# Two dense layers after attention: the up projection as seven half-block products over 768 tokens, with streamed weights

## The chip, the cores and the metric

One NeuronCore of a Trainium2 chip runs the program. The metric is the device time of one execution in microseconds (us). The engines are TensorE (PE, its weight loads are PEld), VectorE (DVE), ScalarE (ACT), GpSimd (POOL) and SyncE (SP, which issues the DMAs here).

## The reference

Attention over 4 x 8 heads of 576 positions and width 64 gives `x`, 2304 tokens by 512. It goes through two dense layers, each an up projection to 2048 and a down projection back to 512, all in float32.

```python
out_up = np.repeat(sm_attn(q_d, k_d, v_d), 4, axis=2)      # attention over positions pooled by 4
out_local = softmax(where(|i - j| < 4, scale * q @ k.T, -1e9)) @ v
x = (out_up + out_local)                                   # 2304 x 512
h = x @ w_in;  g = where(h > 0, h, exp(min(h, 0)) - 1);  x = g @ w_out      # first layer
h = x @ w_in;  r = maximum(h, 0);  g = s * (r * r) + b;  out = g @ w_out    # second layer
```

## The kernel before

**Attention** goes over 16 pairs of heads (4 batches of 4), software-pipelined by hand: `pairs()` runs one `step` per pair on each engine. SP loads queries, keys and values (L240 to L255). GpSimd pools queries and values (L356 to L365) and VectorE keys (L674); VectorE masks, takes maxima, and normalises (L681, L715, L723); ScalarE exponentiates (L555, L565) and copies transposed probabilities out of PSUM (L595 to L605). The result lies in `xy`, with the model dimension on partitions in four groups of 128 (`CH`).

**The dense layers.** Every product is made of three passes: each float32 operand is split into a high part (ScalarE, a copy to fp32r) and a low part (the operand minus its high part), and TensorE adds high x high, high x low and low x high. The tokens go in 6 blocks of 384 (`TB`, `NB`), the inner dimension of 2048 in 16 chunks of 128 (`j`). `up(layer, n, j)` makes one chunk of `h` for one block: 4 groups x 3 passes = 12 matmuls of 384 columns into one of four PSUM banks `ps_h` (L504). `down` adds that chunk's part of the block's output into `ps_y`: in the first layer 12 matmuls of 384 columns (L523), in the second, where tokens lie on output partitions, 9 of 512 columns (L525). TensorE runs `up` two chunks ahead of `down`. Per chunk ScalarE and VectorE apply the activation (first layer: L637, L640, L776; second: L637, L780, L782) and split it (L643 high, L784 low). At the end of a block ScalarE and VectorE copy `ps_y` out (L651, L655, L791, L795); the next block's operand is split four pieces at a time (L576, L729).

**The weights** of a layer stay in SBUF, split once per layer: 256 KB pieces come into the two halves of `wstage` (L263), ScalarE makes the high part (L573, `hi_w`), GpSimd the low part (L370, `lo_w`). Four chunks of the first layer (`win_early`, `wout_early`) are loaded and split during attention; the other twelve (`win_late`, `wout_late`) take the place of attention's buffers. The second layer's weights replace the first's during its last block and the second layer's first. The output goes to memory from `wstage` in pieces of 128 tokens (L317).

The order on every engine is written out in the program; semaphores (`g_ready`, `act_ready`, `w_split`, ...) carry the dependences.

## Time and profile before

| | us |
|---|---|
| median of 3 runs (lowest, highest) | 945.64 (943.05, 947.13) |
| profiled execution: its time | 941.55 |
| profiled execution: span, first to last instruction | 939.7 |
| busy: TensorE matmul, weight load | 907.7, 853.8 |
| busy: VectorE, ScalarE, GpSimd | 412.4, 413.3, 154.2 |
| mean granted TensorE clock | 0.987 of 2.4 GHz |

A span is cut into stretches to see which engine fills which. "Busy" sums the time in which at least one instruction of the engine runs; a matmul's length reaches from its start to its modelled end, and the next one starts before that, so the price of a matmul is the distance between starts. The chain of waits follows the work that ended last back in time, and tells which instructions the time consists of.

### The profile page before, as it was taken

Reading aid. Unit: us, or ns where it says so; the run is one execution under the profiler, and the core shown is the slowest. Engines: PE = TensorE matmul, PEld = TensorE weight load, DVE = VectorE, ACT = ScalarE, POOL = GpSimd, SP = SyncE. Lnnn points to the kernel's source line nnn. Section 1 sums busy time; section 2 is a strip of 40 time slices with the busy share of each in tenths; the row PEclk is TensorE's granted clock in tenths of the full one; section 3 lists DMA queues with packets and bytes.
Section 4 is the critical chain, followed back from the end, with each engine's and each line's share of the span. In section 5 each row is a group of like instructions: output and inputs, shape, how many; then the busy total and the mean of one; then the engine's idle time right before and its main releaser. Section 6 shows DMA issues by size and latency. Waiting matters only on the chain.

```text
span 939.7 us, 16134 instructions
## 1 busy us (share of the span) xinstructions
PE 907.7 (97%) x5936; PEld 853.8 (91%) x5936; DVE 412.4 (44%) x773; ACT 413.3 (44%) x1103; POOL 154.2 (16%) x147
## 2 busy tenths in 40 slices
PE   5988889999999999999999999999999999999998
PEld 4777679999999999999999989989999899899996
DVE  5999964333233233233233353443443443443433
ACT  6888887534334344344366532232232232232222
POOL 6565637500000000000056500000000000000000
PEclk9899999999999999999999999999999999999999
DMA  9999915300000000000044300000000000000000
GB/s 179 181 189 180 178 57 146 101 1 1 1 1 0 0 0 0 0 1 1 1 124 124 90 1 1 34 1 1 34 0 0 34 0 0 34 1 0 35 1 34
DMA packets 42929, 41.47 MB, mean 44 GB/s; under 512 B 3616, under 2 KB 30080, under 8 KB 42880
## 3 DMA queue, kind: packets, MB, share of 16 engines
q1 hardware_dynamic: 42880, 40.83, 19.0%
q8 instruction: 30, 0.49, 0.2%
q14 instruction: 19, 0.16, 0.1%
HBM read 36.09 MB, written 4.72 MB: 43 GB/s over the span
## 4 chain that ended last, share of the span: by engine, by line
PE 87%; DVE 3%; SPq 3%; issue 2%; ACT 2%; DMA 1%; POOL 1%; DVEq 0%; ACTq 0%; POOLq 0%
PE ps_h L504 43%; PE ps_y L525 21%; PE ps_y L523 21%; DMA wstage<-in_w_in 1%; SPq L240 1%; SPq L253 1%; ACT prob L555 1%; DVE stat L704 1%; PE ps_t L437 1%; DVE prob L681 1%; DVE xy L764 1%; SPq L249 1%; DVE kd L674 0%; SPq L254 0%; PE ps_s L413 0%
## 5 line engine op out<-in xcount | busy, mean ns | idle before, releaser
L643 ACT ACTIVATE g_hi<-tmp 128x384 fp32r<-128x384 f32 x192 | 101.0, 526 | 261.9 <-PE ps_y L525 152.2
L784 DVE TENSOR_TENSOR g_lo<-tmp,g_hi 128x384 fp32r<-128x384 f32 x192 | 107.3, 559 | 204.7 <-ACT g_hi L643 204.7
L637 ACT ACTIVATE tmp<-ps_h 128x384 f32<-128x384 f32 x192 | 94.3, 491 | 227.7 <-PE ps_h L504 225.3
L504 PE MATMUL ps_h<-xs_hi,win_late_lo 128*128 128x384 f32 x576 | 193.8, 336 | 0.0
L504 PE MATMUL ps_h<-xs_hi,win_late_hi 128*128 128x384 f32 x576 | 193.8, 336 | 0.0
L504 PE MATMUL ps_h<-xs_lo,win_late_hi 128*128 128x384 f32 x576 | 193.6, 336 | 0.0
L776 DVE SCALAR_TENSOR_TENSOR tmp<-tmp,ps_h 128x384 f32<-128x384 f32 x96 | 53.2, 554 | 161.8 <-ACT tmp L640 161.0
L504 PEld LDWEIGHTS ps_h<-xs_lo,win_late_hi 128*128 128x128 f32 x576 | 108.3, 188 | 3.3
L504 PEld LDWEIGHTS ps_h<-xs_hi,win_late_hi 128*128 128x128 f32 x576 | 108.3, 188 | 3.2
L780 DVE TENSOR_TENSOR tmp<-tmp 128x384 f32<-128x384 f32 x96 | 55.2, 575 | 121.9 <-ACT tmp L637 121.9
L504 PEld LDWEIGHTS ps_h<-xs_hi,win_late_lo 128*128 128x128 f32 x576 | 108.3, 188 | 0.0
L523 PE MATMUL ps_y<-g_hi,wout_late_lo 128*128 128x384 f32 x288 | 96.8, 336 | 0.0
L523 PE MATMUL ps_y<-g_hi,wout_late_hi 128*128 128x384 f32 x288 | 96.8, 336 | 0.0
L523 PE MATMUL ps_y<-g_lo,wout_late_hi 128*128 128x384 f32 x288 | 96.8, 336 | 0.0
L525 PE MATMUL ps_y<-wout_late_hi,g_lo 128*128 128x512 f32 x216 | 85.2, 394 | 0.0
L525 PE MATMUL ps_y<-wout_late_lo,g_hi 128*128 128x512 f32 x216 | 85.0, 394 | 0.0
L525 PE MATMUL ps_y<-wout_late_hi,g_hi 128*128 128x512 f32 x216 | 84.9, 393 | 0.0
L504 PE MATMUL ps_h<-xs_hi,win_early_hi 128*128 128x384 f32 x192 | 64.7, 337 | 0.2 <-DVE xs_lo L729 0.2
L504 PE MATMUL ps_h<-xs_hi,win_early_lo 128*128 128x384 f32 x192 | 64.4, 335 | 0.0
L504 PE MATMUL ps_h<-xs_lo,win_early_hi 128*128 128x384 f32 x192 | 64.3, 335 | 0.0
L370 POOL TENSOR_TENSOR win_early_lo<-wstage,win_early_hi 128x512 fp32r<-128x512 f32 (+1 forms) x8 | 11.1, 1385 | 304.0 <-ACT win_early_hi L573 300.9
L523 PEld LDWEIGHTS ps_y<-g_lo,wout_late_hi 128*128 128x128 f32 x288 | 54.1, 188 | 0.0
(84 smaller groups left out, 1457.7 us busy)
## 6 DMA issues: line engine op xcount, KB each, us to landing
wstage<-in_w_in SPq DMA_DIRECT2D x32, 256.0 KB, 2.7
wstage<-in_w_out SPq DMA_DIRECT2D x32, 256.0 KB, 2.8
qbd<-in_qt SPq DMA_DIRECT2D x32, 144.0 KB, 5.8
kall<-in_kt SPq DMA_DIRECT2D x16, 288.0 KB, 9.7
v<-in_v SPq DMA_DIRECT2D x16, 288.0 KB
out<-wstage SPq DMA_DIRECT2D x18, 256.0 KB, 2.2
vwin<-in_v SPq DMA_DIRECT2D x16, 224.0 KB
vwin<-in_v SPq DMA_DIRECT2D x32, 32.0 KB
```

The lines of the kernel that those rows point to most:

```text
L240: sp.dma_start(qbd[rows, slot, h, :], q_t[bb, 2 * slot + h]).then_inc(qk_loaded[slot], 16)
L249: sp.dma_start(dst[0:QT, 1:NT - 1, :], inner).then_inc(v_loaded[slot], 16)
L253: sp.dma_start(dst[0:QT, t, :], vp[a:a + QT]).then_inc(v_loaded[slot], 16)
L370: pool.tensor_tensor(lo, wstage[slot][:, half, :], hi.bitcast(F32), ALU.subtract).then_inc(w_split[half], 1)
L504: mm = pe.matmul(o, w_chunk(0, a, j)[:, c * P:(c + 1) * P], xs[x][:, slot, c, :], start=(c == 0 and p == 0), stop=(c == CH - 1 and p == 2))
L523: mm = pe.matmul(ps_y[:, c, 0:TB], w_chunk(1, a, j)[:, c * P:(c + 1) * P], g[x][:, j % 2, :], **go)
L525: mm = pe.matmul(ps_y[:, c, 0:DM], g[a][:, j % 2, c * P:(c + 1) * P], w_chunk(1, x, j), **go)
L637: act.activation(x, ps_h[:, j % 4, 0:TB], ACT.Relu, scale=-1.0 if layer == 0 else 1.0).then_inc(relu_ready, 1)
L643: act.activation(g[0][:, j % 2, :], x, ACT.Copy).then_inc(hi_ready, 1)
L776: dve.scalar_tensor_tensor(out=x, in0=x, scalar=-1.0, in1=ps_h[:, j % 4, 0:TB], op0=ALU.add, op1=ALU.max).then_inc(act_ready, 1)
L780: dve.tensor_tensor(x, x, x, ALU.mult).then_inc(square_ready, 1)
L784: dve.tensor_tensor(g[1][:, j % 2, :], x, g[0][:, j % 2, :].bitcast(F32), ALU.subtract).then_inc(g_ready, 1)
```

## The change

The tokens go in 3 blocks of 768 (`TB`), the inner dimension in 8 pairs of chunks; one block and one pair is a **slot** (48 of them, `sl`; `p = sl % 8` is its place in the block). The up projection of a slot is seen as a 2 x 2 block product (halves of the model dimension, halves of the tokens, the two chunks of the pair) and made by **seven products** of half blocks in the manner of Strassen, where there were eight: each product is 2 groups x 3 passes = 6 matmuls of 384 columns into one of now two banks `ps_h`.

- The products need sums: five sums of token quarters per block (`sum_x`, GpSimd, 768 wide, at p = 3, 4, 5 for the next block) and five sums of weight quarters per slot (`sum_w_in`, GpSimd, one operation 512 wide and three 256 wide). All seven operands on each side are split into high and low (`hi_x` ScalarE, `lo_x` VectorE; `hi_w_in` ScalarE, `lo_w_in` GpSimd, 1280 and 512 wide).
- The seven results are put together in `hsum`: three are copied by ScalarE (`copy_product`), VectorE makes two additions in SBUF and six that read PSUM (`add`). The activation then works on 768 columns (`elu_exp`, `elu_max`; in the second layer `relu_square` on VectorE and `affine` on ScalarE), twice a slot, and so does its split (`hi_g`, `lo_g`).
- The weights stay no longer: every slot loads its pair again (two DMAs of 512 KB, laid out on the host so that each partition's part is contiguous), sums and splits it, for every block. GpSimd's waits name what must be free: a slot's sums start when the products of the slot before the last are done.
- The down projection of slot `sl - 1` is cut into 8 units of 6 matmuls (first layer, a 512-column and a 256-column piece per pass) or 6 units of 6 matmuls of 512 columns (second layer), one after each product of slot `sl` from its second on. Its accumulators `ps_y` take six banks. The output goes through `xsum` in six pieces per block.
- In attention the early weight loads and splits are gone; the last pairs have the sums and splits of the first block's operand and of the first slot's weights, and their loads.

```diff
+    TB = 768
+    TH = TB // 2
     NB = TOK // TB
-    W_TURNS = (1, 3)
-    J = F // P
-    STEPS = NB * J
+    FP = w_in0.shape[1]
+    SLOTS = 2 * NB * FP
...
+    ORDER = (1, 2, 3, 6, 5, 4, 7)
+    PROD = len(ORDER)
+    X_SLOT = {k: i for i, k in enumerate(ORDER)}
+    SUMMED = (1, 2, 6, 5, 7)
+    W_SLOT = {6: 0, 7: 1, 1: 2, 3: 3, 4: 4, 2: 5, 5: 6}
+    COPIES = (1, 2, 3, 3, 3, 3, 3)
+    ADDS = (0, 0, 0, 3, 5, 7, 8)
+    NCOPY, NADD = COPIES[-1], ADDS[-1]
...
-        win_early = [keep(f"win_early_{x}", [P, EARLY, CH, P], F32R) for x in ("hi", "lo")]
-        wout_early = [keep(f"wout_early_{x}", [P, EARLY, DM], F32R) for x in ("hi", "lo")]
         xy = keep("xy", [P, CH, TOK])
-        wstage = [keep(f"wstage{i}", [P, 2, DM]) for i in range(2)]
...
+        xsum = keep("xsum", [P, len(SUMMED), 2, TH])
+        xs = [keep(f"xs_{x}", [P, PROD, 2, TH], F32R) for x in ("hi", "lo")]
+        wstage = [keep(f"wstage{i}", [P, 2, 1024]) for i in range(2)]
...
-            win_late = [sbb(f"win_late_{x}", [P, J - EARLY, CH, P], F32R) for x in ("hi", "lo")]
-            wout_late = [sbb(f"wout_late_{x}", [P, J - EARLY, DM], F32R) for x in ("hi", "lo")]
+            wc = [sbb(f"wc_{x}", [P, 2, PROD, KO], F32R) for x in ("hi", "lo")]
+            wsum = sbb("wsum", [P, 5, KO])
+            wo = [sbb(f"wo_{x}", [P, 2, 2, DM], F32R) for x in ("hi", "lo")]
+            g = [sbb(f"g_{x}", [P, 2, 2, TB], F32R) for x in ("hi", "lo")]
+            hsum = sbb("hsum", [P, 2, 2, TB])
+            act_out = sbb("act_out", [P, 2, TB])
+            ps_h = second.enter_context(nc.psum_tensor("ps_h", [P, 2, 512], F32))
+            ps_y = second.enter_context(nc.psum_tensor("ps_y", [P, NO, 512], F32))
...
+            def sum_w_in(sl):
+                pool.wait_ge(w_loaded[0][sl % 2], 16 * (sl // 2 + 1))
+                if sl < 2:
+                    pool.wait_ge(scores_ready, PAIRS)
+                    pool.wait_ge(dscores_ready, PAIRS)
+                else:
+                    pool.wait_ge(prod_ready, PROD * (sl - 1))
+                w = wstage[sl % 2][:, 0, :].rearrange("p (k x) -> p k x", x=KO)
...
+                pool.tensor_tensor(dst[:, 0:2, :], w[:, 0:2, :], w[:, 2:4, :], ALU.add)
+                pool.tensor_tensor(dst[:, 2, :], w[:, 0, :], w[:, 1, :], ALU.add)
+                pool.tensor_tensor(dst[:, 3, :], w[:, 2, :], w[:, 1, :], ALU.subtract)
+                pool.tensor_tensor(dst[:, 4, :], w[:, 3, :], w[:, 0, :], ALU.subtract).then_inc(w_sum, 1)
+            def lo_w_in(sl):
+                pool.wait_ge(w_hi[0], 2 * sl + 2)
+                x = w_part(1, sl, 0, 5)
+                pool.tensor_tensor(x, wsum[:], w_part(0, sl, 0, 5).bitcast(F32), ALU.subtract).then_inc(w_sum_used, 1)
+                w = wstage[sl % 2][:, 0, 0:2 * KO].rearrange("p (k x) -> p k x", x=KO)
+                pool.tensor_tensor(w_part(1, sl, 5, 7), w, w_part(0, sl, 5, 7).bitcast(F32), ALU.subtract).then_inc(w_split[0], 1)
...
+                if 3 <= left <= 7:
+                    if left == 7:
+                        pool.wait_ge(x_ready, 2 * CH + 1)
+                    sum_x(pool, 0, SUMMED[7 - left])
+                if left == 1:
+                    sum_w_in(0)
+                if left == 0:
+                    lo_w_in(0)
             pairs(pool, step)
...
+            for sl in range(SLOTS):
+                blk, p = block_of(sl), sl % FP
+                if sl + 1 < SLOTS:
+                    sum_w_in(sl + 1)
+                if blk + 1 < 2 * NB and 3 <= p <= 5:
+                    if p == 3:
...
+                    for k in SUMMED[2 * (p - 3):2 * (p - 2)]:
+                        sum_x(pool, blk + 1, k)
+                lo_w_out(sl)
+                if sl + 1 < SLOTS:
+                    lo_w_in(sl + 1)
...
+            def product(sl, pos):
+                made = PROD * sl + pos
+                k = ORDER[pos]
+                if pos == 0:
+                    pe.wait_ge(w_split[0], sl + 1)
+                if sl % FP == 0:
+                    pe.wait_ge(x_split, PROD * block_of(sl) + pos + 1)
+                if made < 2:
+                    pe.wait_ge(masked, PAIRS)
+                else:
+                    was, at = divmod(made - 2, PROD)
+                    if at < 3:
+                        pe.wait_ge(h_copied, NCOPY * was + COPIES[at])
+                    else:
+                        pe.wait_ge(h_added, NADD * was + ADDS[at])
+                o = ps_h[:, made % 2, 0:TH]
+                for c in range(2):
+                    for q, (a, x) in enumerate(((0, 0), (0, 1), (1, 0))):
+                        mm = pe.matmul(o, wc[a][:, sl % 2, W_SLOT[k], c * P:(c + 1) * P], xs[x][:, X_SLOT[k], c, :],
+                                       start=(c == 0 and q == 0), stop=(c == 1 and q == 2))
+                mm.then_inc(prod_ready, 1)
...
+            def down(sl, unit):
...
+                if layer == 0:
+                    for q, (a, x) in enumerate(((0, 0), (0, 1), (1, 0))):
+                        for o, start, end in y_pieces(u):
+                            mm = pe.matmul(ps_yf[:, o:o + end - start], wo[a][:, sl % 2, f, u * P:(u + 1) * P],
+                                           g[x][:, sl % 2, f, start:end],
+                                           start=(first and q == 0 and (u % 2 == 0 or end - start == 512)),
+                                           stop=(last and q == 2 and (u % 2 == 1 or end - start == 512)))
+                else:
+                    for m in (2 * u, 2 * u + 1):
+                        for q, (a, x) in enumerate(((0, 0), (0, 1), (1, 0))):
+                            mm = pe.matmul(ps_y[:, m, :], g[a][:, sl % 2, f, m * P:(m + 1) * P], wo[x][:, sl % 2, f, :],
+                                           start=(first and q == 0), stop=(last and q == 2))
...
+            for sl in range(SLOTS):
+                units = 0 if sl == 0 else 2 * CH if layer_of(sl - 1) == 0 else NO
+                done = 0
+                for pos in range(PROD):
+                    product(sl, pos)
+                    if 1 <= pos and done < units and not (sl == SLOTS - 1 and pos in (3, 5)):
+                        down(sl - 1, done)
+                        done += 1
+                for unit in range(done, units):
+                    down(sl - 1, unit)
+            for unit in range(NO):
+                down(SLOTS - 1, unit)
...
+            def copy_product(sl, pos):
+                k = ORDER[pos]
+                r, f = {1: (0, 0), 2: (1, 0), 3: (0, 1)}[k]
+                act.wait_ge(prod_ready, PROD * sl + pos + 1)
+                if sl >= 2:
+                    act.wait_ge(act_ready, 2 * (sl - 2) + 2 - f)
+                act.activation(hsum[:, sl % 2, f, r * TH:(r + 1) * TH], ps_h[:, (PROD * sl + pos) % 2, 0:TH],
+                               ACT.Copy).then_inc(h_copied, 1)
...
+            for sl in range(SLOTS):
+                blk, p = block_of(sl), sl % FP
+                middle = elu_exp if layer_of(sl) == 0 else affine
+                refill = p == FP - 1 and blk + 1 < 2 * NB
+                copy_product(sl, 0)
+                if sl >= 1:
+                    hi_g(sl - 1, 0)
+                if p == 0:
+                    if sl == 0:
+                        hi_x(0, 5)
+                    hi_x(blk, 4)
+                copy_product(sl, 1)
+                if p == 0:
+                    hi_x(blk, 7)
+                hi_w_out(sl)
+                copy_product(sl, 2)
+                if refill:
+                    hi_x(blk + 1, 1)
+                if sl + 1 < SLOTS:
+                    hi_w_in(sl + 1)
+                if refill:
+                    hi_x(blk + 1, 2)
+                middle(sl, 1)
+                if refill:
+                    hi_x(blk + 1, 3)
+                hi_g(sl, 1)
+                if refill:
+                    hi_x(blk + 1, 6)
+                middle(sl, 0)
+                if refill:
+                    hi_x(blk + 1, 5)
+                if p == 0 and blk > 0:
+                    evacuate(blk - 1)
...
+            for sl in range(SLOTS):
+                blk, p, layer = block_of(sl), sl % FP, layer_of(sl)
+                refill = p == FP - 1 and blk + 1 < 2 * NB
+                copied, added = NCOPY * sl, NADD * sl
+                if sl >= 1 and layer_of(sl - 1) == 0:
+                    elu_max(sl - 1, 0)
+                if p == 0:
+                    lo_x(blk, 5)
+                dve.wait_ge(h_copied, copied + 2)
+                dve.tensor_tensor(part(sl, 1, 1), part(sl, 0, 0), part(sl, 1, 0), ALU.subtract).then_inc(h_added, 1)
+                if sl >= 1:
+                    lo_g(sl - 1, 0)
+                if p == 0:
+                    lo_x(blk, 4)
+                dve.wait_ge(h_copied, copied + 3)
+                dve.wait_ge(h_added, added + 1)
+                dve.tensor_tensor(part(sl, 1, 1), part(sl, 1, 1), part(sl, 0, 1), ALU.add).then_inc(h_added, 1)
+                if p == 0:
+                    lo_x(blk, 7)
+                if refill:
+                    lo_x(blk + 1, 1)
+                dve.wait_ge(h_added, added + 2)
+                add(sl, 3, 1, 1, ALU.add)
+                if refill:
+                    lo_x(blk + 1, 2)
+                add(sl, 4, 0, 1, ALU.add)
+                add(sl, 4, 0, 0, ALU.subtract)
+                if layer == 1:
+                    relu_square(sl, 1)
+                add(sl, 5, 1, 0, ALU.add)
+                dve.wait_ge(h_added, added + 5)
+                add(sl, 5, 0, 0, ALU.add)
                 if layer == 0:
-                    dve.wait_ge(elu_exp_ready, t + 1)
-                    dve.scalar_tensor_tensor(out=x, in0=x, scalar=-1.0, in1=ps_h[:, j % 4, 0:TB],
-                                             op0=ALU.add, op1=ALU.max).then_inc(act_ready, 1)
-                else:
-                    dve.wait_ge(relu_ready, t + 1)
-                    dve.tensor_tensor(x, x, x, ALU.mult).then_inc(square_ready, 1)
-                    dve.wait_ge(square_ready, t - STEPS + 1)
-                    dve.tensor_scalar(x, x, sb[:, 0:1], sb[:, 1:2], ALU.mult, ALU.add).then_inc(act_ready, 1)
-                dve.wait_ge(hi_ready, t + 1)
-                dve.tensor_tensor(g[1][:, j % 2, :], x, g[0][:, j % 2, :].bitcast(F32), ALU.subtract).then_inc(g_ready, 1)
-            def evacuate(layer, n, reused):
-                dve.wait_ge(g_used, G_CREDIT + STEPS * layer + J * (n + 1))
-                if layer == 0:
-                    for c in range(2, CH):
-                        dve.tensor_copy(xy[:, c, bass.ds(n * TB, TB)], ps_y[:, c, 0:TB]).then_inc(dve_evac, 1)
-                else:
-                    if reused:
-                        dve.wait_ge(stored[2], 16 * n)
-                    dve.tensor_copy(ostage[2], ps_y[:, 2, 0:DM]).then_inc(dve_evac, 1)
-            layers(dve, chunk, evacuate, split_x)
+                    elu_max(sl, 1)
+                if refill:
+                    lo_x(blk + 1, 3)
+                dve.wait_ge(h_added, added + 7)
+                add(sl, 6, 0, 0, ALU.add)
+                if layer == 1:
+                    relu_square(sl, 0)
+                lo_g(sl, 1)
+                if refill:
+                    lo_x(blk + 1, 6)
+                if p == 0 and blk > 0:
+                    evacuate(blk - 1)
```

**TensorE, the first layer's steady state** (`ps_h<-xs` is an up matmul, `ps_y<-g` a down matmul). Before, from the loop over the blocks, one chunk's up part and then the start of its down part:

```order
L498 REGISTER_ALU [waits w_in_split]
L504 MATMUL ps_h<-xs_hi,win_early_hi 128x384 [waits act_ready]
L504 MATMUL ps_h<-xs_lo,win_early_hi 128x384
L504 MATMUL ps_h<-xs_hi,win_early_lo 128x384
...
L511 REGISTER_ALU [waits w_out_split]
L523 MATMUL ps_y<-g_hi,wout_late_hi 128x384 [waits g_ready]
L523 MATMUL ps_y<-g_lo,wout_late_hi 128x384
```

and of the change, a product and the down unit behind it:

```order
L540 MATMUL ps_h<-xs_hi,wc_hi 128x384 [waits h_added]
L540 MATMUL ps_h<-xs_lo,wc_hi 128x384
L540 MATMUL ps_h<-xs_hi,wc_lo 128x384
...
L568 MATMUL ps_y<-g_hi,wo_hi 128x512 [waits g_ready,w_out_split]
L568 MATMUL ps_y<-g_hi,wo_hi 128x256
L568 MATMUL ps_y<-g_lo,wo_hi 128x512
```

An up part of 12 matmuls with a wait for the activation of four chunks ago has become a product of 6, which waits for the reader of the product before the last.

**GpSimd in the layers.** Before, two chunks of the first layer's late weights (this and its counterpart for the second layer are all its work there):

```order
L370 ISA [waits w_in_hi]
L370 TENSOR_TENSOR win_late_lo<-wstage,win_late_hi 128x512
L370 ISA [waits w_out_hi]
L370 TENSOR_TENSOR wout_late_lo<-wstage,wout_late_hi 128x512
L368 REGISTER_ALU
```

and of the change, slot 3 of a block (other slots have one or none of the `xsum` rows):

```order
L369 TENSOR_TENSOR wsum<-wstage 128x512 [waits w_sum_used,prod_ready,w_in_loaded0]
L370 TENSOR_TENSOR wsum<-wstage 128x256
L371 TENSOR_TENSOR wsum<-wstage 128x256
L372 TENSOR_TENSOR wsum<-wstage 128x256
L216 TENSOR_TENSOR xsum<-xy 128x768 [waits x_split]
L216 TENSOR_TENSOR xsum<-xy 128x768
L387 TENSOR_TENSOR wo_lo<-wstage,wo_hi 128x1024 [waits w_out_hi]
L378 TENSOR_TENSOR wc_lo<-wsum,wc_hi 128x1280 [waits w_in_hi]
L380 TENSOR_TENSOR wc_lo<-wstage,wc_hi 128x512
```

Two operations per chunk in one block of a layer have become seven to nine per slot in all of them.

**VectorE in the first layer.** Before, one chunk:

```order
L776 SCALAR_TENSOR_TENSOR tmp<-tmp,ps_h 128x384 [waits elu_exp_ready]
L784 TENSOR_TENSOR g_lo<-tmp,g_hi 128x384 [waits hi_ready]
```

and of the change, one slot (a slot at the end or the start of a block has `xs_lo` rows between these):

```order
L903 SCALAR_TENSOR_TENSOR act_out<-act_out,hsum 128x768 [waits elu_exp_ready]
L937 TENSOR_TENSOR hsum<-hsum 128x384 [waits h_copied]
L916 TENSOR_TENSOR g_lo<-act_out,g_hi 128x768 [waits hi_ready]
L945 TENSOR_TENSOR hsum<-hsum 128x384 [waits h_added,h_copied]
L896 TENSOR_TENSOR hsum<-hsum,ps_h 128x384 [waits prod_ready,h_added]
L896 TENSOR_TENSOR hsum<-hsum,ps_h 128x384 [waits prod_ready] x3
```

Three operations that take both inputs from SBUF now stand in front of the first addition that empties a bank of `ps_h`.

## Rows read from the trace of the kernel before

**Rows 1.** The page: busy us (share of the span) x instructions, each engine

```profile
PE 907.7 (97%) x5936; PEld 853.8 (91%) x5936; DVE 412.4 (44%) x773; ACT 413.3 (44%) x1103; POOL 154.2 (16%) x147
```

**Rows 2.** Stretches: start:end, length, busy us by engine, clock, DMA share, GB/s

```profile
0.00:133.40 133.40, 106.19 (x1616) 91.23 (x1616) 115.36 (x227) 109.18 (x498) 79.60 (x91) 0.91 0.87 162
133.40:535.00 401.60, 401.40 (x2312) 401.04 (x2310) 128.75 (x232) 191.29 (x380) 72.07 (x55) 1.00 0.13 37
535.00:935.10 400.10, 400.10 (x2012) 361.50 (x2011) 167.62 (x314) 111.70 (x225) 2.58 (x2) 1.00 0.03 11
935.10:939.70 4.60, 0.00 (x0) 0.00 (x0) 0.69 (x1) 1.08 (x2) 0.00 (x0) 1.00 0.46 171
```

**Rows 3.** Chain of waits, longest pieces: start us, us, what; two per layer

```profile
215.45 2.10 PE ps_y L523 x12
...
282.14 2.10 PE ps_y L523 x12
...
611.52 2.09 PE ps_y L525 x9
...
678.33 2.09 PE ps_y L525 x9
```

**Rows 4.** Groups: line engine op, shapes xcount | busy us, mean ns | idle before

```profile
L504 PE MATMUL ps_h<-xs_hi,win_late_hi 128*128 128x384 f32 x576 | 193.8, 336 | 0.0
```

**Rows 5.** Timeline, weight loads and matmuls at the first up matmul: start, length

```profile
133.44 0.19 PEld L504 LDWEIGHTS ps_h<-xs_hi,win_early_hi 128*128 128x128 f32 x1
133.55 0.19 PEld L504 LDWEIGHTS ps_h<-xs_lo,win_early_hi 128*128 128x128 f32 x1
...
133.44 0.44 PE L504 MATMUL ps_h<-xs_hi,win_early_hi 128*128 128x384 f32 x1
133.72 0.34 PE L504 MATMUL ps_h<-xs_lo,win_early_hi 128*128 128x384 f32 x1
```

**Rows 6.** Groups, VectorE, ScalarE and GpSimd, columns as in rows 4

```profile
L784 DVE TENSOR_TENSOR g_lo<-tmp,g_hi 128x384 fp32r<-128x384 f32 x192 | 107.3, 559 | 204.7 <-ACT g_hi L643 204.7
L643 ACT ACTIVATE g_hi<-tmp 128x384 fp32r<-128x384 f32 x192 | 101.0, 526 | 261.9 <-PE ps_y L525 152.2 <-PE ps_y L523 100.8 <-DVE tmp L782 6.3
...
L637 ACT ACTIVATE tmp<-ps_h 128x384 f32<-128x384 f32 x192 | 94.3, 491 | 227.7 <-PE ps_h L504 225.3 <-issue 2.2
...
L776 DVE SCALAR_TENSOR_TENSOR tmp<-tmp,ps_h 128x384 f32<-128x384 f32 x96 | 53.2, 554 | 161.8 <-ACT tmp L640 161.0
...
L370 POOL TENSOR_TENSOR win_late_lo<-wstage,win_late_hi 128x512 f32 x22 | 28.5, 1294 | 33.2 <-ACT win_late_hi L573 33.2
...
L365 POOL TENSOR_TENSOR vd<-v 72x256 f32<-72x256 f32 x16 | 11.6, 726 | 1.3
```

**Rows 7.** Timeline of GpSimd and VectorE at 539 and 75 us; L715 by itself

```profile
539.18 1.29 POOL L370 TENSOR_TENSOR wout_late_lo<-wstage,wout_late_hi 128x512 fp32r<-128x512 f32 x1 [5.17 <-ACT wout_late_hi L573]
...
539.51 1.37 DVE L780 TENSOR_TENSOR tmp<-tmp 128x384 f32<-128x384 f32 x1 [0.34 <-ACT tmp L637]
...
75.75 3.48 DVE L715 TENSOR_TENSOR prob<-prob,stat 128x630 f32<-128x630 f32 x1
...
76.20 1.26 POOL L370 TENSOR_TENSOR wout_early_lo<-wstage,wout_early_hi 128x512 f32 x1
77.42 1.14 POOL L356 TENSOR_TENSOR q_half<-qbd 128x576 f32<-128x576 f32 x1
...
L715 DVE TENSOR_TENSOR prob<-prob,stat x16: 815/942/3478, 17.0 to 126.7; 128x630 f32<-128x630 f32 x16
```

**Rows 8.** DMA issues (KB each, us to landing); SP's last issues in the timeline

```profile
wstage<-in_w_in SPq DMA_DIRECT2D x32, 256.0 KB, 2.7
...
935.90 1.50 SPq L317 DMA_DIRECT2D out<-wstage  x3
```

**Rows 9.** Timeline of GpSimd and ScalarE at the end of attention

```profile
125.05 0.73 POOL L365 TENSOR_TENSOR vd<-v 72x256 f32<-72x256 f32 x1
...
129.83 0.59 ACT L595 ACTIVATE probt<-ps_t 70x512 f32<-70x512 f32 x1 [0.73 <-PE ps_t L437]
```

456 lines of the change are left out of this document (226 added, 230 removed).

## The prediction

> **What bounds the kernel now.** I read the page's busy line and the table of stretches first. TensorE is busy 97% of the span [rows 1]; by stretch [rows 2] it is full from 133.4 us to 935.1 us, the two dense layers, while VectorE and ScalarE are busy a third to a half of that stretch and GpSimd hardly. Only the first 133.4 us (attention, DMA engines 0.87 busy) and the last 4.6 us (stores) are something else. In the chain of waits, one block of 384 tokens recurs every 66.69 us in the first layer and every 66.81 us in the second [rows 3], with nothing but matmuls in it. A first-layer block has 16 x 24 = 384 matmuls of 384 columns: **0.1737 us each**. A second-layer block has 192 of those and 144 of 512 columns: (66.81 - 33.35)/144 = **0.2324 us each**. (The 336 ns of the group [rows 4] are from start to drain, and overlap; the spacing is the price.) So time saved on TensorE counts in full, as long as the other engines keep up.
>
> **The sum**, against the profiled execution (span 939.7 us, time 941.55 us; the median of the runs shown is 945.64 us, 4.1 us more).
>
> *Matmuls.* 768 tokens by 256 inner columns used to take 48 up matmuls of 384 columns, and now take 7 products x 2 halves x 3 passes = 42. The down part keeps its columns: 24 x 512 and 24 x 256 in the first layer, 36 x 512 in the second. Per pair of chunks ("slot"): 42 x 0.1737 + 24 x (0.2324 + 0.116) = 15.66 us, and 42 x 0.1737 + 36 x 0.2324 = 15.66 us. 48 slots make 751.7 us where 801.7 stood: **-50.0 us**.
> The 256-column matmul (576 of them) is in no row. I price it in proportion, 0.116 us (256/384 of 0.1737 and 256/512 of 0.2324 agree). What could hold it up is the weight load of 128 columns in front of each. After the one idle moment at 133.44 two loads start 0.11 us apart, and the second matmul starts 0.28 us after the first, that is one load plus one 384-column matmul [rows 5]: a load takes about 0.108 us, just under 0.116. From below, then, 0.116; from above 0.174, if nothing goes faster than what was seen in the layers: +33 us. I take 0.116, with 0.12 as likely (+2).
> A rule that would make the gain smaller: the Trainium skill ("TensorE: Matmul & The Clock Gate", section Back-to-back issue gap) gives about 131 ns per 512-column matmul as the sustained spacing. By it the 288 matmuls saved would be worth at most 38 us; this trace shows 232 ns, and the trace decides.
>
> *VectorE and ScalarE.* A slot now asks of VectorE six adds that read PSUM, two of 384 columns wholly in SBUF, and four of 768 in SBUF. From 0.559 and 0.554 us at 384 [rows 6] (384 columns at 0.96 per ns plus 0.16) a 768-wide one costs 0.96: 8 x 0.56 + 4 x 0.96 = 8.3 us of 15.7. ScalarE: 3 copies of 0.49, six passes of 768 (four in the second layer) at 0.85, by 0.526 at 384 [rows 6] and 1.2 columns per ns, and the weights at the same rate, 1.05 + 1.9: 9.5 us. Both fit. Per block, seven operand splits of 768 come on top on each, in the last slot of a block and the first of the next; five in the last make 13.7 us on ScalarE.
>
> *GpSimd and the lock.* GpSimd now sums and splits all weights again for each of the six blocks. A 512-wide operation takes 1.29 us and a 256-wide one 0.73 [rows 6]. 4096 elements a slot: 10.0 to 10.4 us, plus 5 operand sums of 1.9 per block, **about 11.4 us** a slot. Alone that fits too. But VectorE operations with both inputs in SBUF don't run beside GpSimd's: at 539.51 a squaring of normally 0.56 us takes 1.37, ending 0.41 us after the GpSimd operation that had begun before it (539.18 + 1.29); at 75.75 one that takes 0.82 at its shortest takes 3.48, while two whole GpSimd operations pass it [rows 7]. The additions that read PSUM (L776) keep their 554 ns. Per slot the operations concerned hold VectorE for about 2 x 0.35 + 4 x 0.75, with 0.65 for the operand splits, 4.3 us. 11.4 + 4.3 = **15.7 us, just what TensorE needs**. That is no room at all, but not over it either.
> The Trainium skill ("SBUF — State Buffer", section Who interferes with whom) states this as an exclusive lock on a port pair that the two engines share, the later one fully blocked; the trace agrees, at 1.37 against 0.56 us.
> Where does it hurt? A product's PSUM bank (there are two now, four before) must be read within 3.15 us of the product's end in the first layer, 3.8 in the second. The third of VectorE's SBUF operations in a slot stands in front of the add that frees the bank of product 4; in ordinary slots that add is done 1.7 us early by my count. In slots 3 and 4 of a block GpSimd has two operand sums as well, its 1024-wide operation blocks VectorE from about 6.6 to 9.0 us into the slot, and the add is 0.6 to 1 us late. In the last slot the second operand split waits for the 1280-wide operation and product 7 is 1.4 us late; in the first slot of the next block three splits do the same, 2.5 us; the copy out of the down banks then costs up to 0.5. That is 6 us a block at five block borders in the first layer; the second has 0.7 us more slack each time. From below 0 (all of it inside the slack), from above 40 us (8 a block); I take **+18 us**.
>
> *Weights by DMA.* 512 KB pieces, 1 MB a slot, 67 GB/s, against 162 moved in attention [rows 2]. 256 KB land in 2.7 us [rows 8], so 512 KB in about 5; they are issued over 12 us before they are needed. Nothing, unless the SP queue is held by a store, which is issued a slot late on purpose.
>
> *Into the layers.* About 1 MB of weights no longer stands in front of the last attention loads: at 162 to 180 GB/s up to -6 us, but VectorE is busy 0.86 of that stretch, so I take -3 (0 to -6). Then GpSimd sums the first weights after its last attention work (ends 125.8 [rows 9]): to about 130.5 with the lock; ScalarE splits them, to 132.5, in front of the copy that was at 129.83 [rows 9], so the last pair is 2.5 us later; GpSimd's split (4.3 us) ends at 137. First product at about 137 in place of 133.4: +4. Together **+1**.
> Slot 0 has no down work to hide behind, two banks, and the operand splits of products 5 to 7 in line with the copies: about 10.7 us for 7.3 of work, and then slot 1's weights are late (GpSimd: 3.5 + 2.6 + 4.3 and the lock), at about 14. +6.7; the wait may lower the granted clock as attention's gaps did (mean 0.91 [rows 2]), +1.3: **+8**.
> *Out of them.* Six banks and six stores in place of three: the three issues take 1.50 us [rows 8] and the last landed 4.6 us after the matmuls [rows 2]; three more at 0.6, and 1.5 MB at some 200 GB/s: **+3.5**.
>
> Sum: -50.0 + 18 + 1 + 8 + 3.5 = **-19.5 us**, span 920, profiled time 922, median **926 us**.
>
> **The rivals.** (No change is here within 0.5%, 941 to 950 us, about what a measurement can tell.)
> *A, all covered:* waits at block borders stay within the slack, +3 in place of +18: **911 us**. For it: ordinary slots have 1.7 us to spare. Against: the 15.7 us of the two engines together.
> *B, GpSimd and VectorE in turn become the bound:* one mechanism, the lock, and one point: if the two together need over 16.4 us a slot, the -50 is used up (37 us left after start and end, over 48 slots = 0.78). With whole durations, 11.6 + 5.8 = 17.4 us, the layers take 835 us: -50 + 84 + 12.5 = +46, **992 us, slower**. For it: the 3.48 us row, where VectorE missed two turns. Against: at 539.51 it got the first, and start-up and tail of an operation run outside the lock.
> *C, the same lock, but not past that point* (16.4 a slot, +35 in place of +18): **943 us**, no change.
> *D, a 256-column matmul costs 0.174 us:* +33, **959 us**, slower. Against: the 0.11 us between two loads.
> That the change does not do what it says: the order of TensorE's instructions has 42 for 48 up matmuls, so it does.
>
> **How the numbers follow.** Forecast 0.47 (own range 914 to 938), A 0.27, C and what lies near it 0.13, B 0.09, D 0.04. Faster: the first two and half of C's share, 0.81; same 0.08; slower 0.11. The range leaves out B and D and A's lower end: **905 to 944 us**.
>
> **What would show it.** After: 2016 up matmuls; 0.174 and 0.232 us spacing, 0.116 to 0.12 for 256 columns (wrong if 0.17). First product near 137 us and slot 1 starting 14 us later. Slots of 15.7 us in the middle of blocks, with 1 to 3 us more in slots 3, 4, 7 and 0. TensorE's waits for h_added longer than those for weights; if it waits for the input weights' split in every slot, B is right. VectorE's SBUF operations of 0.56 us at 1 to 3 us, PSUM adds at 0.55. Tail of 8 us. The prediction is wrong if slots average over 16.3 us, or if no block border costs anything.

## The result and the profile after

The changed kernel takes **991.5 us** (median of 4 runs, 990.1 to 994.5) against 945.3 us of the kernel before (4 runs, 943.1 to 947.1): a ratio of 1.049, 95% interval 1.046 to 1.053. It is slower, by 46 us where 19.5 us less were forecast. (A few executions of the variants below took over 1.5% longer than the fastest of the same kernel; the ratios leave them out, the medians don't.) The page's line of busy times, which answers to [rows 1]:

```profile
PE 888.9 (90%) x5648; PEld 795.8 (81%) x5648; DVE 768.6 (78%) x866; ACT 538.5 (54%) x1078; POOL 728.8 (74%) x449
```

TensorE has less to do and waits more; VectorE went from 412 to 769 us, GpSimd from 154 to 729. The table of stretches, as in [rows 2], cut at the first up matmul, at the change of layers and at the last matmul:

```profile
0.00:145.80 145.80, 107.49 (x1616) 91.60 (x1616) 125.19 (x228) 109.80 (x493) 86.23 (x95) 0.89 0.75 149
145.80:568.10 422.30, 392.18 (x2153) 361.85 (x2154) 329.51 (x324) 236.25 (x325) 339.26 (x188) 0.97 0.21 62
568.10:981.80 413.70, 389.21 (x1881) 342.33 (x1879) 312.03 (x313) 190.91 (x259) 303.34 (x168) 0.98 0.21 63
981.80:988.40 6.60, 0.05 (x1) 0.00 (x0) 1.89 (x3) 1.57 (x3) 0.00 (x0) 0.65 0.64 238
```

The first product starts at 145.9 us (133.4 before), the layers last 836.0 us (801.7), the end 6.6 us (4.6), and in the layers the clock is no longer 1.00. The matmuls keep their prices (starts 0.174 us apart for 384 columns, 0.231 for 512, 0.117 for 256): 751.7 us of work, and 84.3 us of something else. The distance from slot to slot, taken between the first up matmuls of each, tells where it lies. In the first layer a block reads, in us: **24.4**, 15.7, 15.7, 16.5, 17.1, 18.2, 15.7, 16.8. In the second: **22 to 24**, 17.3, 16.2, 16.2, 17.0, 17.0, 16.2, 16.2. Over 15.66 us each the five first slots of blocks make 39.2 us, the slots with operand sums (p = 3 to 5) 22.5, the last ones 4.5, the rest 8.0, together 74.2; slot 0 is 17.5 us long for 7.3 of work, 10.2. (The 17.3 is of blocks 4 and 5, in block 3 that slot takes 15.7; the last block has no operand sums, and its slots 3 to 5 take 16.2.)

The groups of instructions on the page (columns as in rows 4):

```profile
L540 PE MATMUL ps_h<-xs_hi,wc_hi 128*128 128x384 f32 x672 | 235.1, 350 | 41.4 <-DVE hsum L896 38.9
L896 DVE TENSOR_TENSOR hsum<-hsum,ps_h 128x384 f32<-128x384 f32 x288 | 148.6, 549 | 85.3 <-PE ps_h L540 83.2
L945 DVE TENSOR_TENSOR hsum<-hsum 128x384 f32<-128x384 f32 x48 | 113.9, 2373 | 16.1 <-ACT hsum L699 16.0
L378 POOL TENSOR_TENSOR wc_lo<-wsum,wc_hi 128x1280 fp32r<-128x1280 f32 x48 | 153.3, 3194 | 14.2 <-ACT wc_hi L635 14.0
```

and of VectorE alone, further down:

```profile
L845 DVE TENSOR_TENSOR xs_lo<-xsum,xs_hi 128x768 fp32r<-128x768 f32 x30 | 59.3, 1985 | 0.2 <-ACT xs_hi L628 0.2
L937 DVE TENSOR_TENSOR hsum<-hsum 128x384 f32<-128x384 f32 x48 | 38.1, 793 | 66.4 <-ACT hsum L699 66.4
```

L896, an add with one operand in PSUM, takes 549 ns as forecast. L945, the same size with both operands in SBUF, takes 2373 ns on average. It stands in VectorE's program in front of the adds that free the product banks, and TensorE's largest wait (38.9 us) is for those. The first slot of block 1 in the timeline, VectorE, then GpSimd, then TensorE:

```profile
287.20 0.95 DVE L845 TENSOR_TENSOR xs_lo<-xy,xs_hi 128x768 fp32r<-128x768 f32 x1
288.07 2.77 DVE L945 TENSOR_TENSOR hsum<-hsum 128x384 f32<-128x384 f32 x1
290.76 3.63 DVE L845 TENSOR_TENSOR xs_lo<-xsum,xs_hi 128x768 fp32r<-128x768 f32 x1
294.31 1.47 DVE L896 TENSOR_TENSOR hsum<-hsum,ps_h 128x384 f32<-128x384 f32 x3
...
287.58 2.85 POOL L387 TENSOR_TENSOR wo_lo<-wstage,wo_hi 128x1024 fp32r<-128x1024 f32 x1 [4.56 <-ACT wo_hi L644]
290.39 3.19 POOL L378 TENSOR_TENSOR wc_lo<-wsum,wc_hi 128x1280 fp32r<-128x1280 f32 x1
...
295.00 0.66 PE L540 MATMUL ps_h<-xs_hi,wc_hi 128*128 128x384 f32 x1 [4.56 <-DVE hsum L896]
```

VectorE is blocked twice in a row: L945 ends 0.41 us after GpSimd's L387, when L378 has already begun in the record, and the next one 0.81 us after L378 (whole operations of 0.56 and 0.95 us took 2.77 and 3.63), and TensorE stands still for 4.56 us. Then the granted clock falls, in two stretches of equal length:

```profile
294.40:301.20 6.80, 6.20 (x20) 5.94 (x21) 3.27 (x6) 2.53 (x3) 1.12 (x1) 0.50 0.27 80
301.20:308.00 6.80, 6.80 (x40) 6.24 (x40) 4.96 (x7) 4.48 (x9) 4.10 (x4) 1.00 0.00 0
```

At 0.50, the lower level of 1.2 GHz, 20 matmuls start in 6.8 us, at 2.4 GHz 40: some 3.4 us more. The two borders behind it look the same; at the last two, where 3.15 us instead of 5.0 lie between two matmuls' starts, the clock is down for 3.4 us. 4.6 and 3.4 are 8 of the 8.8 us that this slot takes too long. From 145.8 to 981.8 us, 39.2 us are at the lower level (12.0 in slot 0, the rest at the borders), with TensorE busy in 34.7 of them: by an estimate from these, half of it, some 17 of the 84.3 us, is the clock's.

### The profile page after: what moved, and what is told of

It is laid out like the page before. It is cut to its first block, busy times and chain, and to the rows that moved or that the text cites. A ratio compares the mean times of both kernels' runs of the same rounds, so it can differ in the third digit from the quotient of the medians.

```text
span 988.4 us, 15290 instructions
## 1 busy us (share of the span) xinstructions
PE 888.9 (90%) x5648; PEld 795.8 (81%) x5648; DVE 768.6 (78%) x866; ACT 538.5 (54%) x1078; POOL 728.8 (74%) x449
## 4 chain that ended last, share of the span: by engine, by line
PE 58%; DVE 28%; issue 8%; ACT 3%; POOL 2%; DVEq 0%; ACTq 0%; POOLq 0%
PE ps_h L540 26%; PE ps_y L568 15%; PE ps_y L575 14%; DVE xs_lo L845 5%; DVE hsum L945 4%; DVE act_out L910 4%; DVE hsum L896 3%; DVE g_lo L916 3%; DVE stat L818 1%; DVE prob L795 1%; PE ps_s L440 1%; DVE prob L829 1%; ACT xs_hi L628 1%; DVE xy L883 1%; DVE stat L812 1%
## 5 line engine op out<-in xcount | busy, mean ns | idle before, releaser
L540 PE MATMUL ps_h<-xs_hi,wc_hi 128*128 128x384 f32 x672 | 235.1, 350 | 41.4 <-DVE hsum L896 38.9
L540 PE MATMUL ps_h<-xs_lo,wc_hi 128*128 128x384 f32 x672 | 231.2, 344 | 0.0
L540 PE MATMUL ps_h<-xs_hi,wc_lo 128*128 128x384 f32 x672 | 230.9, 344 | 0.0
L896 DVE TENSOR_TENSOR hsum<-hsum,ps_h 128x384 f32<-128x384 f32 x288 | 148.6, 549 | 85.3 <-PE ps_h L540 83.2
L387 POOL TENSOR_TENSOR wo_lo<-wstage,wo_hi 128x1024 fp32r<-128x1024 f32 x48 | 133.8, 2788 | 72.1 <-ACT wo_hi L644 72.1
L540 PEld LDWEIGHTS ps_h<-xs_hi,wc_hi 128*128 128x128 f32 x672 | 129.9, 193 | 58.8 <-DVE xs_lo L845 28.4
L378 POOL TENSOR_TENSOR wc_lo<-wsum,wc_hi 128x1280 fp32r<-128x1280 f32 x48 | 153.3, 3194 | 14.2 <-ACT wc_hi L635 14.0
L916 DVE TENSOR_TENSOR g_lo<-act_out,g_hi 128x768 fp32r<-128x768 f32 x96 | 138.0, 1438 | 6.1 <-ACT g_hi L729 5.4
L540 PEld LDWEIGHTS ps_h<-xs_lo,wc_hi 128*128 128x128 f32 x672 | 130.1, 194 | 8.4
L540 PEld LDWEIGHTS ps_h<-xs_hi,wc_lo 128*128 128x128 f32 x672 | 129.8, 193 | 0.0
L945 DVE TENSOR_TENSOR hsum<-hsum 128x384 f32<-128x384 f32 x48 | 113.9, 2373 | 16.1 <-ACT hsum L699 16.0
```

The source lines that it names most:

```text
L378: pool.tensor_tensor(x, wsum[:], w_part(0, sl, 0, 5).bitcast(F32), ALU.subtract).then_inc(w_sum_used, 1)
L387: pool.tensor_tensor(x, wstage[sl % 2][:, 1, :], hi.bitcast(F32), ALU.subtract).then_inc(w_split[1], 1)
L540: mm = pe.matmul(o, wc[a][:, sl % 2, W_SLOT[k], c * P:(c + 1) * P], xs[x][:, X_SLOT[k], c, :], start=(c == 0 and q == 0), stop=(c == 1 and ...
L896: dve.tensor_tensor(o, o, ps_h[:, (PROD * sl + pos) % 2, 0:TH], op).then_inc(h_added, 1)
L916: dve.tensor_tensor(g[1][:, sl % 2, f, :], act_out[:, f, :], g[0][:, sl % 2, f, :].bitcast(F32), ALU.subtract).then_inc(g_ready, 1)
L945: dve.tensor_tensor(part(sl, 1, 1), part(sl, 1, 1), part(sl, 0, 1), ALU.add).then_inc(h_added, 1)
```

## The experiments

Three theories. **L**: the lock of GpSimd and VectorE costs time because the locked instructions stand in VectorE's program ahead of the adds on which TensorE waits. **T**: the two in turn simply have more work than a slot has time (rival B of the prediction). **V**: VectorE has too much work of its own. "Excess" is what slots 0 to 46 take over 15.66 us each; the time is the median of a kernel's runs, the rest is from the one profiled execution.

| | time, us | ratio to before (95%) | first product | first slots of blocks | ordinary, 2nd layer | excess |
|---|---|---|---|---|---|---|
| changed kernel | 991.5 | 1.049 (1.046 to 1.053) | 145.9 | 24.4, 22.1 | 16.2 | 76.0 |
| e1 GpSimd light | 936.0 | 0.990 (0.987 to 0.994) | 145.9 | 15.7, 15.7 | 15.7 | 22.3 |
| e2 narrow | 960.2 | 1.017 (1.009 to 1.025) | 146.6 | 19.1, 16.6 | 16.3 | 42.9 |
| e3 adds from PSUM | 946.6 | 1.001 (0.998 to 1.004) | 147.4 | 18.5, 17.7 | 16.2 | 30.4 |
| e4 later split | 972.6 | 1.029 (1.020 to 1.037) | 143.6 | 19.4, 18.9 | 16.2 | 56.9 |
| e5 all three | 953.8 | 1.010 (1.007 to 1.012) | 151.8 | 18.0, 19.2 | 16.2 | 35.5 |
| e6 light in attention | 981.9 | 1.042 (1.035 to 1.049) | 132.0 | 24.2, 22.1 | 16.2 | 75.2 |
| e7 sums on VectorE | 990.2 | 1.049 (1.047 to 1.052) | 142.0 | 24.4, 22.1 | 16.2 | 75.5 |
| e8 e5 and swap | 961.4 | 1.019 (1.017 to 1.022) | 144.2 | 18.0, 19.3 | 16.2 | 44.8 |
| e9 e3 and late sums | 941.1 | 0.997 (0.993 to 1.000) | 134.8 | 18.5, 17.7 | 16.2 | 32.3 |
| e10 e9 and g order | 958.1 | 1.019 (1.014 to 1.024) | 135.5 | 18.6, 22.3 | 16.2 | 53.1 |
| e11 late sums alone | 983.0 | 1.040 (1.036 to 1.045) | 136.7 | 24.2, 22.1 | 16.2 | 77.2 |
| e12 e9 and border | 946.5 | 1.003 (1.000 to 1.006) | 138.5 | 19.1, 18.2 | 16.2 | 39.7 |
| e13 e12 and deferred | 932.0 | 0.989 (0.986 to 0.992) | 132.6 | 19.1, 18.2 | 15.7 | 26.9 |
| e14 e9 and deferred | 930.8 | 0.985 (0.980 to 0.990) | 135.2 | 18.5, 17.7 | 15.7 | 21.2 |

(The two numbers for first slots are blocks 1 to 3 and blocks 4 and 5.)

**e1: GpSimd light.** The weights' sums and low parts are 8 columns wide from slot 2 on: this kernel leaves most of their work out. The code shows the sums; `lo_w_in` and `lo_w_out` are cut in the same way.

```diff
+                if sl >= 2:
+                    pool.tensor_tensor(dst[:, 4, 0:8], w[:, 3, 0:8], w[:, 0, 0:8], ALU.subtract).then_inc(w_sum, 1)
+                    return
...
```

> GpSimd's sums and low parts of the weights are 8 columns wide instead of 256 to 1280 from slot 2 on (their work is left out, all waits stay). Theory L (a VectorE operation with both inputs in SBUF waits for GpSimd's long operations): those operations fall back to 0.56 us (384 wide) and 0.96 us (768 wide), the first slot of a block to about 17 us from 24.4, the others to 15.7, and the time to 920 us (911 to 930). Theory V (VectorE's own 8.3 us a slot and two PSUM banks are too much, the lock is a side show): no less than 970 us.

55 us come back, the first slots fall to 15.7 us. VectorE executes the same 866 instructions, so V is out. In the groups of this kernel:

```profile
L955 DVE TENSOR_TENSOR hsum<-hsum 128x384 f32<-128x384 f32 x48 | 30.9, 644 | 30.9 <-ACT hsum L709 30.9
L855 DVE TENSOR_TENSOR xs_lo<-xsum,xs_hi 128x768 fp32r<-128x768 f32 x30 | 31.8, 1064 | 5.5 <-ACT xs_hi L638 5.3
```

These are L945 and L845 of the changed kernel: 0.64 instead of 2.37 us, 1.06 instead of 1.99. The time expected was 16 us too low: 12 of them are the attention, which this run doesn't touch, and four second-layer slots still took 18 to 20 us, waiting for `g_lo`. L and T both allow this result.

**e2: narrow.** GpSimd's 1280-wide operation is cut into 512, 512 and 256, the 1024-wide one into two; same columns.

```diff
-                pool.tensor_tensor(x, wsum[:], w_part(0, sl, 0, 5).bitcast(F32), ALU.subtract).then_inc(w_sum_used, 1)
+                for a, z in ((0, 2), (2, 4), (4, 5)):
+                    ins = pool.tensor_tensor(w_part(1, sl, a, z), wsum[:, a:z, :], w_part(0, sl, a, z).bitcast(F32), ALU.subtract)
+                ins.then_inc(w_sum_used, 1)
```

> GpSimd's 1280-wide operation is cut in 512, 512, 256 and the 1024-wide one in two of 512: the same columns, more points at which VectorE can get in. Theory L in its form 'one long operation at the wrong moment': VectorE's wait per operation is at most 1.3 us, the first slot of a block falls from 24.4 to about 19, the time to 955 us (940 to 970). Theory T (the two engines in turn need more than a slot in all, as the rival of the prediction had it): the same work, the same time, 988 to 995 us.

960.2 us: 31 us less with the same work (and three more starts a slot on GpSimd). T expected nothing, and GpSimd was even busy longer in the layers (674 us against 643). How long one turn lasts counts. But the sum isn't free of limits: in the slots with two operand sums (p = 4, 17.9 us) TensorE now waited for the weights' low part, 8.6 us in five waits, which is rival B's sign.

**e3: adds from PSUM.** VectorE's two SBUF sums of a slot (L937, L945) read their second operand from the product's bank, while ScalarE's copy of it is made all the same; the bank is free one wait later.

```diff
-                dve.tensor_tensor(part(sl, 1, 1), part(sl, 1, 1), part(sl, 0, 1), ALU.add).then_inc(h_added, 1)
+                dve.tensor_tensor(part(sl, 1, 1), part(sl, 1, 1), ps_h[:, (PROD * sl + 2) % 2, 0:TH], ALU.add).then_inc(h_added, 1)
```

(L937 likewise, and `product` waits for `h_added` instead of `h_copied` at two places)

> The two additions of the results of products 1 to 3 read the second one's input from its PSUM bank instead of its copy in SBUF, behind the copy; product 4 and 5 wait for them. They no longer need the lock. Theory L: L945 (2.37 us on average now) takes 0.55, slots 3 to 5 of a block fall by 0.8 to 2.5 us each to 15.7, the first slot of a block still has its third operand split in the way and falls by 2 to 3: 965 us (955 to 975). Theory T: only 2 x 0.35 us a slot leave the lock, 975 to 985 us, spread evenly over the slots. Theory V: no change, 988 to 995.

946.6 us, better than L hoped. GpSimd's program is untouched, the ordinary slots of the first layer and those with operand sums all take 15.73 us, and after its first 4.0 us in the layers TensorE's clock stays at 2.4 GHz to the last matmul:

```profile
PE 875.3 (93%) x5648; PEld 783.9 (83%) x5648; DVE 658.5 (70%) x866; ACT 537.7 (57%) x1078; POOL 716.3 (76%) x449
...
L947 DVE TENSOR_TENSOR hsum<-hsum,ps_h 128x384 f32<-128x384 f32 x48 | 26.4, 550 | 17.6 <-ACT hsum L701 17.6
```

The sum that took 2373 ns takes 550 with an operand in PSUM. 45 us for taking 96 of VectorE's instructions out of the lock, with GpSimd's work as it was: **T falls** as the cause of these 45 us, L stands.

**e4: later split.** The low parts of operands 7, 1 and 2 stand behind the adds of product 5 instead of ahead of those of product 4.

```diff
-                if p == 0:
-                    lo_x(blk, 7)
-                if refill:
-                    lo_x(blk + 1, 1)
...
                 add(sl, 4, 0, 0, ALU.subtract)
+                if p == 0:
+                    lo_x(blk, 7)
+                if refill:
+                    lo_x(blk + 1, 1)
+                    lo_x(blk + 1, 2)
```

> VectorE's operand splits 7 (first slot of a block) and 1 and 2 (last slot) move behind the additions that free the banks of products 4 and 5; nothing is left out. Theory L, with the order of VectorE's work as what turns a lock wait into a TensorE wait: the first slot of a block loses its idle time of 4.5 us and with it the half clock of 6.8 us (3.4 us): 24.4 to about 17, five times, 955 us (945 to 965). Theory T: the splits take as long as before, the same total, 985 to 995 us.

972.6 us: 19 us back where 35 were expected. The first slots go from 24.4 to 19.4 us, the slots with operand sums don't get shorter (that of p = 5 got 1.5 us longer in two blocks). There L945 itself stands in the way; this run alone doesn't show that, e3 does.

**e5: all three together.**

> The three partial remedies together (sums read from the bank behind the copy, late low parts, narrow GpSimd instructions). Lock-in-the-chain theory: each of the three took away part of the same wait, so together they do not add up (44.9 + 31.3 + 18.9 us would be 95, more than the 84 us by which the layers exceed their matmuls), but block-first slots should fall from 18.5 us (adds alone) towards 16.5 and the others stay at 15.73; the first product still comes at 144 to 148 us and ordinary slots of the second layer at 16.2. Time 935 us (925 to 945). Rival, that what is left of the excess is VectorE's own load and not the lock: no better than the adds alone, 944 to 950 us.

Missed, by the forecast and by its rival: 953.8 us, 7 more than e3 alone. The first slots of blocks 1 to 3 are 18.0, but the first product came at 151.8, and in the second layer the first two slots of a block lost what others gained. GpSimd is busy 653 us in these layers, 628 in e3's, and TensorE waited once, 2.5 us, for the weights' low part; that the narrow instructions are what costs here was not tested by itself.

**e6 and e7: attention.** In the changed kernel VectorE is blocked there too. VectorE, then GpSimd, in the timeline:

```profile
91.20 4.02 DVE L829 TENSOR_TENSOR prob<-prob,stat 128x630 f32<-128x630 f32 x1
...
90.97 0.72 POOL L355 TENSOR_TENSOR vd<-v 72x256 f32<-72x256 f32 x1
91.65 1.80 POOL L216 TENSOR_TENSOR xsum<-xy 128x768 f32<-128x768 f32 x1
93.41 1.14 POOL L346 TENSOR_TENSOR q_half<-qbd 128x576 f32<-128x576 f32 x1
```

and by line, all sixteen instances (shortest/median/longest ns), one of three columns and one that reduces:

```profile
L812 DVE TENSOR_SCALAR stat<-stat x16: 165/669/3544, 12.7 to 135.7; 96x3 f32<-96x3 f32 x16
...
L803 DVE TENSOR_REDUCE stat<-prob x16: 810/811/812, 9.9 to 126.8; 128x9 f32<-128x630 f32 x16
```

L829 (0.82 us when free) ends 0.67 us after the third GpSimd operation. The new operand sum L216 stands between two operations that GpSimd had before. e6 makes the first block's operand sums 8 columns wide (it leaves their work out); e7 makes them whole, on VectorE, in the same pairs.

```diff
-                    sum_x(pool, 0, SUMMED[7 - left])
+                    sum_x(dve, 0, SUMMED[7 - left])
```

> The operand sums of the first block, which GpSimd makes between the last attention pairs, are 8 columns wide instead of 2 x 384 (their work is left out; the sums' tile is filled with zeros at the program's start instead). The rest is the changed kernel. Theory S, that these five GpSimd instructions and the VectorE instructions of the attention that wait behind them cost the 12 us between 133.4 and 145.9 us: first product at 136 to 139 us, time 982 us (979 to 986). Rival W, that the first weights' sums and low parts at the attention's end cost it (VectorE's normalise at 130.1 us took 4.3 us behind them, and the low part waited 7.7 us at 141.7): first product not before 143 us, time 988 to 992 us.

> The same five operand sums are whole but made by VectorE, behind the normalising of the next pair, instead of by GpSimd. By S the lock goes and five VectorE instructions of about 1 us come in: first product at 138 to 142 us, time 984 us (981 to 989). If VectorE's own load were the limit of the attention (theory V), five more instructions on it make it later: first product at 146 us or later, 991 us or more.

e6: first product at 132.0, 13.9 us earlier and 4 earlier than S expected, the layers unchanged: rival W is out, the sums are what makes this profile's attention longer. The time is less clear: the four lie in two pairs, 975 and 988 us, one on either side of S's range, and the profile is of the lower pair. That their median, 981.9, meets the forecast is luck, and no trace shows what the upper pair did. e7: 142.0 in the profile, but 990.2 us, nothing gained. The stretch from 60 to 120 us says why (kernel before, changed, e7):

```profile
60.00:120.00 60.00, 49.78 (x784) 42.79 (x783) 57.72 (x112) 49.72 (x238) 37.52 (x36) 0.91 0.96 176
```
```profile
60.00:120.00 60.00, 44.09 (x657) 37.39 (x657) 56.50 (x96) 41.32 (x197) 36.09 (x33) 0.83 0.87 181
```
```profile
60.00:120.00 60.00, 48.02 (x771) 40.95 (x770) 58.56 (x107) 46.98 (x223) 31.07 (x30) 0.91 0.93 179
```

VectorE is busy 94 to 98% of it in each, so work or a wait laid on it there has no idle time to go into. In the changed kernel it gets 96 instructions through where it had got 112. TensorE's clock is lower there too, 0.83 against 0.91, and no run tells what part of the 12 us that is.

**e11: late sums.** VectorE makes three sums in the last pair but one (`left == 1`) and two behind the attention, where it has idle time; GpSimd's go. ScalarE's high parts of operands 1 and 2 move one pair back with them, which the code below leaves out, so the run tests the two together.

```diff
+                if left == 1:
+                    dve.wait_ge(x_ready, 2 * CH + 1)
+                    for k in (1, 2, 6):
+                        sum_x(dve, 0, k)
...
             lo_x(0, 6)
+            sum_x(dve, 0, 5)
+            sum_x(dve, 0, 7)
```

> The changed kernel with the first block's operand sums made by VectorE where it has idle time, three in the attention's last pair but one and two behind the attention, instead of by GpSimd between the last pairs. Making them on VectorE in the same pairs as before gained nothing in the time (990.2 us), and VectorE is 96 to 98% busy there before and after. Theory S2, that VectorE binds the attention until the last two pairs, so that any work or lock wait laid on it there comes on top, but not behind: first product at 134 to 138 us, time 982 us (978 to 986). Rival, that what is late is the end of the attention itself (the weights' sums and the operands' splitting): first product at 142 us or later, 988 to 992.

> The same move of the operand sums, on top of the kernel whose VectorE reads the bank behind the copy (946.6 us, first product 147.4). If the two costs are separate, the gain of the move is the same there: first product at 134 to 139 us, layers as before it (790 us from the first product to the last matmul), time 936 us (931 to 941). If the gain in the attention is given back in the first slots, because GpSimd's weight sums are then what the second slot waits for: 942 to 947.

First product at 136.7 (e11) and, on top of e3, 134.8 (e9). In all six profiles with late sums (e9 to e14) it comes at 132.6 to 138.5 us, in all seven with GpSimd's at 143.6 to 151.8. 983.0 and 941.1 us: the gain is 8.5 and 5.5 us, separate from that in the layers; both ranges of times are wide (e9: 934.5 to 952.5).

**e8, e10, e13: the half microsecond of the second layer.** Its ordinary slots take 16.2 us in every kernel so far but e1. Of e9, VectorE and TensorE at the start of such a slot:

```profile
572.50 1.19 DVE L913 SCALAR_TENSOR_TENSOR act_out<-hsum 128x768 f32<-128x768 f32 x1
573.62 1.49 DVE L919 TENSOR_TENSOR g_lo<-act_out,g_hi 128x768 fp32r<-128x768 f32 x1
...
575.25 0.48 PE L573 MATMUL ps_y<-wo_hi,g_hi 128*128 128x512 f32 x1 [0.31 <-DVE g_lo L919]
```

The first down product waits for `lo_g(sl, 1)`, which stands behind the squaring of the other half. e8 swaps the two (on e5). e10 swaps them on e9 and moves the previous half's `hi_g` and `lo_g` one copy and one sum back. e13 moves also the affine of half 0 into the next slot behind the first copy, for p = 0 to 5 (on e12).

```diff
+        def deferred(sl):
+            return sl >= NB * FP and sl % FP <= 5
...
                 copy_product(sl, 0)
+                if sl >= 1 and deferred(sl - 1):
+                    affine(sl - 1, 0)
...
                 copy_product(sl, 1)
+                if sl >= 1 and deferred(sl - 1):
+                    hi_g(sl - 1, 0)
...
                 lo_g(sl, 1)
+                if deferred(sl):
+                    relu_square(sl, 0)
```

> As the three remedies together, and in the second layer VectorE makes g's low part (hidden half 1) before the squaring of half 0 instead of behind it. In the trace of the changed kernel's variant, the first down product of each second-layer slot started 0.5 us late behind that low part, and the slots took 16.23 us where those of the first layer took 15.73. If that order is the cause: ordinary slots of the second layer 15.7 us, 22 slots x 0.5 = 11 us below the three remedies together, 924 us (915 to 935). Rival, that the high part before it (ScalarE's) is late as well and the low part gains nothing: within 3 us of the three remedies together.

> As the kernel with late sums, and in the second layer VectorE makes g's low part (half 1) ahead of the squaring of half 0, with the high and low part of the previous slot's half 0 moved behind the second copy and the second add, so that nobody waits for the delayed squaring there. The swap alone moved the 0.5 us per slot from the down product (which had waited for g's low part) to the third up product (which then waited for ScalarE's copy behind g's high part): slots stayed at 16.21. If the order of the engines' programs is the cause of the 0.5 us: ordinary second-layer slots 15.7 us, 11 us below the kernel with late sums, 925 us (920 to 932). If it is the sum of work on VectorE or GpSimd in such a slot: 16.2 again, within 3 us of it.

> As the one with the operand parts out of the way, and in 18 slots of the second layer the squaring of half 0 stands behind g's low part of half 1, and everything that follows from it (the affine, the high and the low part of half 0) stands in the next slot behind the first copy, the second copy and the second sum. The earlier move left ScalarE's affine of that half ahead of the next slot's first copy, where it waited for the delayed squaring. If the order of the programs costs the 0.5 us: the slots 1 to 6 of the second layer's blocks take 15.7 us instead of 16.2, 8 to 9 us less than without it, 924 us (918 to 930). If it is load: 16.2 and the same time within 3 us.

e8 and e10 missed, and are 8 and 17 us slower than what they stand on. The idle moment only moved, to the third product of a slot, which then waited for ScalarE's copy: ScalarE stood at the affine of the half whose squaring had been put off. Slots at the block borders of the second layer became up to 6 us longer. e13 moves the follow-up on every engine, and the ordinary slots fall to 15.68 us as expected (those with two operand sums only to 16.0 to 16.2). Its gain, 14.6 us, is more than the 8 to 9 expected: in the profiles 12.8 are in the excess, and the first product came 6 us earlier, which the edit doesn't touch. So the order is enough to end the half microsecond. It is the lock's too: at 572.50 and 573.62 the two operations take 1.19 and 1.49 us for 0.95, and in e1, without GpSimd's weight work, these slots take 15.7 us in the old order.

**e12: the border.** On e9: ScalarE's high part of operand 4 behind the second copy, VectorE's low parts of 4 and 7 behind the second sum and the adds of product 5.

```diff
-                    hi_x(blk, 4)
                 copy_product(sl, 1)
                 if p == 0:
+                    hi_x(blk, 4)
                     hi_x(blk, 7)
```

> The kernel with late sums, and in the first slot of a block the operand parts make way for the product's sums: ScalarE makes the high part of operand 4 behind the second copy instead of ahead of it, VectorE the low part of 4 behind the second sum and that of 7 behind the fifth. In the trace without this, two products of such a slot started 1.55 and 1.15 us late, behind just these instructions. If their order is the cause: block-first slots 16.0 to 17.0 us instead of 18.5 and 17.7, five of them, 8 us less, 933 us (928 to 937). If the lock is (the low parts take 2 to 3 us wherever they stand, and the last products wait for them instead): 18 us or more, 939 to 943.

The rival was right about the slot, 19.1 us instead of 18.5; the time, 946.5, is above even its range. Two late products became four, 0.4 to 0.8 us each; in this slot the low parts still take 2.3 to 2.4 us wherever they stand:

```profile
277.24 2.41 DVE L841 TENSOR_TENSOR xs_lo<-xy,xs_hi 128x768 fp32r<-128x768 f32 x1
...
280.96 2.32 DVE L841 TENSOR_TENSOR xs_lo<-xsum,xs_hi 128x768 fp32r<-128x768 f32 x1
```

**e14: what helped, together.** e3's sums, late operand sums and the deferred squaring.

> Adds from the bank, late operand sums and the deferred squaring, without the reordering of the operand parts at the block borders, which had made the block-first slots 0.5 us longer. Sum: 941.1 us for the first two, less 18 slots x 0.5 = 9 us for the third, 932 (926 to 936); or from the other side 932.0 us less five borders x 0.6 = 929. Block-first slots 18.5 and 17.7, slots 1 to 6 of the second layer 15.7. If the gains are not separate, the freed time is lost at the borders again: 19 us or more there, 936 to 941.

930.8 us as expected, ratio to before 0.985 (0.980 to 0.990): it is faster than both kernels, though by only 1.5% than the one before. Its busy line and its layers:

```profile
PE 867.1 (94%) x5648; PEld 780.6 (85%) x5648; DVE 670.1 (73%) x871; ACT 537.1 (58%) x1078; POOL 717.5 (78%) x444
```
```profile
135.20:916.40 781.20, 762.92 (x4034) 691.88 (x4032) 552.90 (x638) 426.42 (x582) 642.08 (x355) 1.00 0.23 67
```

GpSimd works 642 us in the layers, as in the changed kernel (642.6), and they take 781 us instead of 836, at a granted clock of 1.00. Nothing of GpSimd's work in the layers was removed or made smaller; only what VectorE does in the lock, and the order on VectorE and ScalarE, have changed.

## Why the prediction was wrong

Against the profiled execution the sum was -19.5 us and came out as +48.7 (spans 939.7 and 988.4). The slots average 17.4 us (836.0/48), past the 16.3 that the prediction named as a sign of being wrong. Term by term:

- *Matmuls, -50.0:* held. 2016 up matmuls, spacings as forecast, the 256-column one at 0.117 us, so rival D is out.
- *Waits at block borders, +18:* measured **74.2**. This is the step that failed, in two ways. First, the length of a run of blocked operations: it had each of them late by itself and most of it inside the slack. In the trace one blocked VectorE operation ends when the next GpSimd operation has already begun, so the one behind it is blocked as well: 2.77 and 3.63 us in a row, 4.9 us more than the two need alone. Unblocked, in e1, the same add was done 1.7 us before the sixth product could start (281.59 and 283.31); here VectorE was already 1.4 us later against TensorE when the run began, which left 0.3. "The first slot of the next block, 2.5 us" was 8.8. Second, it priced the wait but not its consequence: at the borders these waits were followed by 6.8 us (at the last two borders 3.4) at the lower clock, that is 3.4 and 1.7 us more. The forecast had this only for slot 0. And slots 3 to 5 of a block were 0.8, 1.4 and 2.5 us late, not 0.6 to 1 in two of them.
- *GpSimd, 11.4 us a slot, 15.7 with VectorE's share:* measured 642.6/48 = 13.4 us of GpSimd alone. Its three 256-wide sums take 1.44, 1.43 and 0.83 us instead of 0.73. With VectorE's 4.3 that would be 17.7 us, longer than a slot; e14 has the same 13.4 us and slots of 15.7. The two don't simply add: what the 256-wide sums take beyond 0.73 is their own wait for VectorE, so that time stands in both terms. The sum was not what set the time of these slots, though e2 shows that GpSimd is near its limit.
- *Into the layers, +1:* measured **+12.4**. The five operand sums between the last pairs had no price. VectorE "is busy 0.86 of that stretch" was used for the DMA term alone, and it is the mean of the whole attention; from 60 to 120 us it was 57.7 of 60. Without the sums there the first product came 13.9 us earlier in the profile of e6, 9.1 in that of e11, and the times fell by 9.6 and 8.5 us.
- *Slot 0, +8:* 10.2, near by number and not by mechanism: slot 1's weights were ready 14.0 us after the first product, as forecast, but slot 0 itself took 17.5, with 5.3 us of waiting for VectorE's add and 12.0 us at the lower clock where 1.3 us of loss had been counted. *Out of them, +3.5:* 2.0. *Weights by DMA, 0:* held; no matmul group names a DMA.

**Rival B** gave 992 us and 835 us for the layers; measured are 991.5 and 836.0. The numbers agree and the mechanism doesn't: in the layers TensorE waited only once, 0.5 us, for the weights' split, which was named as B's sign, and 38.9 us for `h_added`, and the point of 16.4 us a slot decides nothing (e3, e14). That the lock would decide was right; the chance of 0.09 was too low: B was the only case in which the lock costs the whole gain, and the forecast's own rows (a 3.48-us VectorE operation behind two GpSimd ones, [rows 7]) had said that one blocked operation can lose 2.7 us, more than the 1.7 of slack that was counted for the whole chain.

By the Trainium skill ("SBUF — State Buffer", section Who interferes with whom) a VectorE instruction with at most one SBUF input, outside the two-port modes, stays out of the lock, and a reduction never enters it on this chip. The runs agree: 550 ns against 2373 for the same sum with and without an operand in PSUM (e3), and 810 to 812 ns for all sixteen reductions of L803. The condition on the modes matters: L812 has one input, in SBUF, and was blocked for up to 3.5 us.

## What to carry to other kernels

When work is laid on an engine that shares a lock with another, price the longest run of blocked instructions in the chain that the bottleneck waits for, not the sum per period; then see which of them can have an operand in PSUM instead (45 us here for two operand expressions). The sum per period still has to fit: e2's slots with two operand sums waited for GpSimd. Read each engine's busy share in the stretch where the work is put, not over the stage: an engine at 96% for 60 us has no room for more. And when an order of instructions is changed to end a wait, move what follows from it on all engines, or the wait reappears on the next one's program, as it did twice here.

## What the runs showed of the hardware

- Small instructions wait as long as large ones: L812, a scalar operation on 3 columns, took 165 ns at its shortest and 3544 at its longest, in the changed kernel's attention. The longest began 0.08 us after a GpSimd operation and ended with the third.
- VectorE can miss several turns: while GpSimd's operations follow one another without a gap, a waiting instruction got in only behind the second or third (4.02 us at 91.20).
- GpSimd is slowed by the lock as well: in the changed kernel's layers a sum of 256 columns took 1.44 to 1.55 us when a VectorE operation with both inputs in SBUF was under way at its start, and 0.72 to 0.75 otherwise (L370 to L372; 0.73 in [rows 6]).
- In the layers of the changed kernel, 5.0 us between two matmuls' starts were followed by 6.8 us at 1.2 GHz three times, 3.15 us by 3.4 us twice; 2.6 us twice by none. These figures are no limit: in e2 eight starts were 2.3 us apart, three of them followed by 3.4 us at 1.2 GHz and five by none. e3, e9 and e14 begin the layers with 3 to 4 us at 1.2 GHz, left from the attention's end, and then show 2.4 GHz to the last matmul.

What stays open: which order would end the 17.7 to 18.5 us of the first slots of blocks (e1's 15.7 show that they come from GpSimd's work on the weights, e12 only that one other order doesn't help), and why single runs of one kernel differ by up to 18 us (e9: 934.5 to 952.5). That the attention falls into one of two lengths is a guess from e6's two pairs of times.
